# Output of a second feed-forward network with token rows: the hidden tile held, 384 and 192 weight columns moving

## The chip, the cores and the metric

One core of a Trainium2 chip runs the kernel. The metric is the device time of one execution in microseconds, median of several runs. The engines are TensorE (PE, with its weight loads as PEld), VectorE (DVE), ScalarE (ACT), GpSimd (POOL) and SyncE (SP), which issues most DMAs.

## The reference

Eight thousand tokens of 192 channels pass three stages:

```python
# causal mixing, per head: softmax over 7 taps, weighted sum of the last 7 tokens
out = np.einsum('hk,bskhg->bshg', w, x_unf)
# network 1: 192 -> 1536 -> 192
g = x @ w_gate; silu = g / (1 + np.exp(-g)); val = x @ w_val
x = silu * val @ w_out1
# network 2: 192 -> 2048 -> 192
h = x @ w_in
g = np.where(h > 0, h, np.exp(np.minimum(h, 0)) - 1)
out = g @ w_out2          # the stage that the change touches
```

All inputs and outputs are float32: x is (2, 4096, 192), the output (8192, 192).

## The kernel before

The tokens are worked off in 16 chunks of T = 512. Inside the chip everything is channel-major: channels (or hidden units) on the 128 partitions, tokens along the columns. Matmuls use rounded f32 (F32R); to keep f32 accuracy every operand is split into a high part and the rest, a low part, and a product is the sum high x high, low weights x high data and high weights x low data.

A chunk passes two phases. `mix_phase(n)` projects the mixed chunk n into gate and value tiles (12 inner tiles f), and in between runs `down1`, the output of network 1, three tiles behind. `elu_phase(n)` does the same for network 2: 8 iterations j project two of the 16 inner tiles k = 2j, 2j+1, and `down2` follows 4 tiles (LAG2, two iterations) behind; tiles 12 to 15 of a chunk are taken in the first two iterations of the `mix_phase` after the next. So TensorE's program alternates one projection (18 matmuls) with two `down` tiles (20 matmuls). Chunks 2 to 14 are a hardware loop (`Fori`), in which wait values are registers; the others are written out.

All these matmuls use half of the 128 rows of the array, 64 rows deep. They are issued in twos: one on the upper rows (TOP, partitions 0 to 63), one on the lower (LOW), with different weights and different PSUM banks, and the two run side by side.

`down(w, ...)` holds 128 weight columns and moves 512 tokens. Its 192 output channels are a main part of 128 (banks `MAIN_A` from the upper rows, `MAIN_B` from the lower) and a tail of 64. The tail's 64 columns of high weights and 64 of low weights share one 128-column tile `tails`, which gives `TAIL_A` and `TAIL_B`. Per inner tile these are five pairs of matmuls: three with `hid_hi`, two with `hid_lo`:

```python
both(MAIN_A, MAIN_B, main_hi, hi, a, False)
both(MAIN_A, MAIN_B, main_lo, hi, False, False)
both(TAIL_A, TAIL_B, tails, hi, a, False)
pe.wait_ge(lo_sem, lo_count)
both(MAIN_A, MAIN_B, main_hi, lo, False, z)
return both(TAIL_A, TAIL_B, tails, lo, False, z)
```

The hidden tile comes from a chain over the engines: VectorE takes the minimum (L837), ScalarE the exponential (L632), VectorE makes `hidden` (L855), ScalarE its rounded high part `hid_hi` (L647), GpSimd the rest `hid_lo` (L460). `hid_hi` and `hid_lo` are rings of 4 tiles; ScalarE may write one when `down2_done` says that `down2` of four tiles before is through. The banks of the projections are used again after two iterations, when `elu_done` has come.

After the 16th tile the output z of a chunk has to leave its four banks. At f == 1 of the later `mix_phase`, ScalarE copies `TAIL_A` and `MAIN_A` (`copy_z`, L584 and L585), VectorE `TAIL_B` and `MAIN_B` (L759, L760); `down1` of the next chunk waits for the copies. GpSimd adds the halves (`sum_z_tail`, `sum_z_main`, f == 2 and 3), SyncE moves the lower half of the tail to the upper partitions by a DMA (`swap_z`), GpSimd adds that (`fold_z_tail`, f == 6), and VectorE transposes main and tail in blocks of 32 x 32 (`turn_z`, L766 and L769, f == 10 and 11). SyncE then stores six bands of 32 channels (`store_band`, 64 KB each, runs of 128 bytes). SyncE's queue in the loop is `swap_halves(n)`, `load_x(n + 3)`, `cross1(n + 1)`, `swap_z(n - 1)`, `cross2(n)`, `store(n - 1)`, all in order.

The end is written by hand: `last_blocks` orders the last four tiles so that the tails finish first, uses all 128 rows for the main parts of tiles 14 and 15, and folds the tail with one more matmul (`FOLDED`); `finish` on VectorE adds and transposes, and SyncE and ScalarE store three bands each.

## Time and profile before

| what | value |
|---|---|
| time, median of 3 runs | 1212.76 us (1210.73 to 1216.68) |
| profiled execution, its own time | 1211.81 us |
| its span, first to last instruction | 1209.9 us |
| TensorE busy | 1202.1 us, 99% |
| TensorE weight loads busy | 1034.7 us, 86% |
| VectorE / ScalarE / GpSimd busy | 878.5 / 669.6 / 767.1 us |
| granted TensorE clock | 1.0 |

Busy time of an engine is the union of its instructions' records. A matmul's record is longer than its share of the engine, since matmuls overlap: records of 0.39 us follow each other in twos. The timeline merges equal instructions that follow each other; "x6" are six of them, and the start is that of the first. A bracket gives the idle time before a row and what ended it. "PEld" is the weight load that belongs to a matmul; a wait of TensorE sits at the load.

### The profile page before, as it was taken

What the parts mean: (1) busy time and instruction counts of PE and PEld (TensorE: products, weight loads), DVE (VectorE), ACT (ScalarE), POOL (GpSimd) and SP (SyncE); (2) the same over time, 40 slices, a digit from 0 to 9 for tenths busy, and PEclk for the clock granted to TensorE, in tenths of its full rate; (3) what the DMA queues carried; (4) which work ended last, traced back from release to release, by engine and by line L of the source; (5) the groups of instructions that cost most, each with busy time, mean ns of one, the idle gap of its engine ahead of it and who ended that gap; (6) DMA issues with size and microseconds to landing.
All of it is one profiled execution on the core that took longest, in us unless ns stands there. A gap on an engine that the chain in (4) does not pass through costs nothing.

```text
span 1209.9 us, 28143 instructions
## 1 busy us (share of the span) xinstructions
PE 1202.1 (99%) x10274; PEld 1034.7 (86%) x10274; DVE 878.5 (73%) x1180; ACT 669.6 (55%) x1081; POOL 767.1 (63%) x576
## 2 busy tenths in 40 slices
PE   9999999999999999999999999999999999999998
PEld 6999888888888888888888888888888888888886
DVE  7788675886758777686776868768687675886776
ACT  6556555464554645546465554655646555465564
POOL 7787755576655756657665576655656655666565
PEclk9999999999999999999999999999999999999999
DMA  8412011120111202012020120201202011120101
GB/s 180 117 40 45 15 34 33 33 46 22 35 23 33 43 22 41 20 30 43 22 48 22 22 43 22 56 13 22 43 22 56 13 30 35 27 51 21 24 19 31
DMA packets 147343, 45.27 MB, mean 37 GB/s; under 512 B 126512, under 2 KB 136368, under 8 KB 147312
## 3 DMA queue, kind: packets, MB, share of 16 engines
q1 hardware_dynamic: 145200, 44.27, 17.8%
q10 hardware_dynamic: 2112, 0.59, 0.2%
q8 instruction: 20, 0.33, 0.1%
q14 instruction: 11, 0.09, 0.0%
HBM read 16.12 MB, written 6.29 MB: 19 GB/s over the span
## 4 chain that ended last, share of the span: by engine, by line
PE 97%; DVE 1%; POOL 1%; issue 0%; ACT 0%; DVEq 0%; ACTq 0%
PE up L928 54%; PE down L928 42%; POOL hid_lo L460 1%; DVE mixed L898 0%; DVE hidden L855 0%; DVE act L837 0%; POOL up_w_lo L334 0%; ACT L656 0%; POOL y_main L464 0%; POOL halves L464 0%; PE down L1129 0%; DVE mixed L895 0%; DVE taps_head L881 0%; DVE stage L766 0%; DVE stage L781 0%
## 5 line engine op out<-in xcount | busy, mean ns | idle before, releaser
L460 POOL TENSOR_TENSOR hid_lo<-hidden,hid_hi 128x512 fp32r<-128x512 f32 x447 | 608.6, 1374 | 426.9 <-ACT hid_hi L613 255.9
L928 PE MATMUL down<-hid_hi,out_w 64*128 64x512 f32 x2684 | 393.0, 391 | 0.0
L928 PEld LDWEIGHTS down<-hid_hi,out_w 64*128 64x128 f32 x2684 | 270.9, 185 | 43.2 <-issue 0.8
L928 PE MATMUL down<-hid_lo,out_w 64*128 64x512 f32 x1790 | 288.7, 391 | 0.0
L798 DVE TENSOR_TENSOR hidden<-act,up 128x512 f32<-128x512 f32 x191 | 130.5, 683 | 168.3 <-ACT act L596 166.8
L837 DVE TENSOR_SCALAR act<-up 128x512 f32<-128x512 f32 x256 | 164.9, 686 | 105.7 <-PE up L928 105.7
L928 PE MATMUL up<-in_b_hi,up_w_lo 64*128 64x512 f32 x1128 | 231.6, 391 | 0.0
L928 PE MATMUL up<-in_b_lo,up_w_hi 64*128 64x512 f32 x1128 | 231.6, 391 | 0.0
L928 PE MATMUL up<-in_b_hi,up_w_hi 64*128 64x512 f32 x1128 | 231.6, 391 | 0.0
L613 ACT ACTIVATE hid_hi<-hidden 128x512 fp32r<-128x512 f32 x192 | 121.6, 633 | 187.6 <-DVE hidden L798 187.5
L632 ACT ACTIVATE act<-act 128x512 f32<-128x512 f32 x256 | 157.5, 633 | 97.6 <-DVE act L837 96.5
L647 ACT ACTIVATE hid_hi<-hidden 128x512 fp32r<-128x512 f32 x256 | 158.6, 630 | 94.4 <-DVE hidden L855 91.1
L928 PEld LDWEIGHTS down<-hid_lo,out_w 64*128 64x128 f32 x1790 | 181.4, 185 | 28.3
L730 DVE SCALAR_TENSOR_TENSOR mixed<-x_t,taps,mixed 128x512 f32<-128x512 f32 x192 | 205.5, 1109 | 0.0
L596 ACT ACTIVATE act<-up 128x512 f32<-128x512 f32 x191 | 114.3, 599 | 140.0 <-PE up L928 136.5
L855 DVE SCALAR_TENSOR_TENSOR hidden<-act,up 128x512 f32<-128x512 f32 x256 | 168.9, 680 | 29.3 <-POOL hid_lo L460 21.2
L928 PE MATMUL up<-in_a_hi,up_w_hi 64*128 64x512 f32 x786 | 161.6, 392 | 0.2 <-DVE hidden L855 0.2
L928 PE MATMUL up<-in_a_hi,up_w_lo 64*128 64x512 f32 x786 | 161.4, 391 | 0.0
L928 PE MATMUL up<-in_a_lo,up_w_hi 64*128 64x512 f32 x786 | 161.4, 391 | 0.0
L928 PEld LDWEIGHTS up<-in_b_lo,up_w_hi 64*128 64x128 f32 x1128 | 115.2, 185 | 17.8
L928 PEld LDWEIGHTS up<-in_b_hi,up_w_hi 64*128 64x128 f32 x1128 | 115.2, 185 | 17.8
L928 PEld LDWEIGHTS up<-in_b_hi,up_w_lo 64*128 64x128 f32 x1128 | 115.2, 185 | 17.8
(103 smaller groups left out, 810.8 us busy)
## 6 DMA issues: line engine op xcount, KB each, us to landing
x_raw<-x_dram SPq DMA_DIRECT2D x136, 64.0 KB, 2.2
out_dram<-stage SPq DMA_DIRECT2D x93, 64.0 KB, 1.8
in_b_hi<-in_b_hi SPq DMA_DIRECT2D x32, 128.0 KB, 2.3
in_b_lo<-in_b_lo SPq DMA_DIRECT2D x32, 128.0 KB, 2.3
swapped<-halves SPq DMA_DIRECT2D x32, 128.0 KB, 2.3
in_a_hi<-in_a_hi SPq DMA_DIRECT2D x30, 128.0 KB, 2.3
in_a_lo<-in_a_lo SPq DMA_DIRECT2D x30, 128.0 KB, 2.3
stage<-w_out_dram SPq DMA_DIRECT2D x7, 384.0 KB, 3.9
```

The lines of the kernel that those rows point to most:

```text
L460: return pool.tensor_tensor(hid_lo[:, slot, :], hidden[:, s, :], hid_hi[:, slot, :].bitcast(F32), ALU.subtract)
L596: nc.scalar.activation(act[:, f % 2, :], gate_bank(f, n)[:, :], ACT.Silu)\
L613: nc.scalar.activation(hid_hi[:, f % RING, :], hidden[:, f % 2, :], ACT.Copy)\
L632: nc.scalar.activation(act[:, k % 2, :], act[:, k % 2, :], ACT.Exp).then_inc(exp_done, 1)
L647: nc.scalar.activation(hid_hi[:, k % RING, :], hidden[:, k % 2, :], ACT.Copy)\
L730: v.scalar_tensor_tensor(mixed[:, part, :], src, tap, mixed[:, part, :], ALU.mult, ALU.add).then_inc(mix_step, 1)
L798: v.tensor_tensor(hidden[:, f % 2, :], act[:, f % 2, :], val_bank(f, n)[:, :], ALU.mult)\
L837: v.tensor_scalar(act[:, k % 2, :], elu_bank(k)[:, :], 0.0, None, ALU.min)\
L855: v.scalar_tensor_tensor(hidden[:, k % 2, :], act[:, k % 2, :], -1.0, elu_bank(k)[:, :], ALU.add, ALU.max).then_inc(elu_done, 1)
L928: return nc.tensor.matmul(dst, lhsT, rhs, start=start, stop=stop, skip_group_check=True)
```

## The change

Network 2's output is computed the other way round. The hidden tile is held and the weights move: 128 tokens of `hid_hi` or `hid_lo` are the held operand, and the columns that move are 384 (192 high and 192 low weights) for `hid_hi` and 192 (high) for `hid_lo`. The result has tokens as rows. Each of the four banks holds one block of 128 tokens: columns 0 to 191 high weights, columns 192 to 383 low weights times high data.

The upper and the lower rows now add into the same banks, at different times: while the upper rows write block b, the lower write `b_low`. Two inner tiles are taken together, in four turns for the high part and four for the low part. Two turns later rows and banks are exchanged, and TensorE waits on its own semaphore `z_turn` for the end of the matmuls two turns before.

```diff
-            def down2(m, k):
...
-                down(out2_w[:, k, :], k % RING, k == 0, False, lo2_done, N2 * m + k + 1)\
-                    .then_inc(down2_done, 1)
+            def by_tokens(k, data, b, b_low, first=False, last=False):
+
+                w = out2_w[:, k, 0:2 * D] if data is hid_hi else out2_w[:, k, 0:D]
+                cols = slice(0, 2 * D) if data is hid_hi else slice(0, D)
+                start, stop = first and b in (0, 1), last and b in (0, 1)
+                mm(Z[b][:, cols], data[TOP, k % RING, b * P:b * P + P], w[TOP], start, stop)
+                return mm(Z[b_low][:, cols], data[LOW, k % RING, b_low * P:b_low * P + P], w[LOW], start, stop)
+
+            def down2_pair(m, k0):
+                two = (k0, k0 + 1)
+                turns = 4 * (N2 // 2 * m + k0 // 2)
...
+                for turn, (b, b_low) in enumerate(((0, 2), (1, 3), (2, 0), (3, 1))):
+                    if turn >= 2:
+                        pe.wait_ge(z_turn, turns + turn - 1)
+                    for k in two:
+                        pe.wait_ge(hi2_done, N2 * m + k + 1)
+                        end = by_tokens(k, hid_hi, b, b_low, first=k == 0)
+                    if turn < 2:
+                        end.then_inc(z_turn, 1)
+                for turn, (b, b_low) in enumerate(((3, 1), (2, 0), (1, 3), (0, 2))):
+                    if turn >= 2:
+                        pe.wait_ge(z_turn, turns + turn + 1)
+                    for k in two:
+                        pe.wait_ge(lo2_done, N2 * m + k + 1)
+                        end = by_tokens(k, hid_lo, b, b_low, last=k == N2 - 1)
+                    if turn < 2:
+                        end.then_inc(z_turn, 1)
+                end.then_inc(down2_done, 2)
```

`down1` keeps its form; its first tile waits for `result_done` of the last block in place of `z_a` and `z_b`. ScalarE copies the four blocks' low products into `result`, VectorE adds the high ones to them, at the same places where the four copies stood; halves, swap, fold and transposes are gone from GpSimd, SyncE and VectorE. A chunk is stored in one DMA, each row of 768 bytes whole. The low weights of `w_out2` are made in one operation for each piece where there were two.

```diff
+                for b in range(BLOCKS):
+                    nc.scalar.activation(result[:, b, :], Z[b][:, D:2 * D], ACT.Copy).then_inc(z_a, 1)
...
+            def add_z(m):
+                for b in range(BLOCKS):
+                    v.wait_ge(z_a, BLOCKS * m + b + 1)
+                    v.tensor_tensor(result[:, b, :], result[:, b, :], Z[b][:, 0:D], ALU.add)                        .then_inc(result_done, 1)
...
-                for q in range(OUT_BANDS):
-                    store_band(sp, m, q)
+                store_tokens(sp, m)
```

The end: tiles 12 and 13 are a `down2_pair`; tiles 14 and 15 use all 128 rows, one block after the other, and each block is copied, added and stored alone.

```diff
+                down2_pair(CHUNKS - 1, N2 - 4)
+                for b in (0, 1):
+                    for k in two:
+                        whole(b, k, hid_hi)
+                    whole(b, N2 - 2, hid_lo)
+                for b in (0, 1):
+                    whole(b, N2 - 1, hid_lo, True).then_inc(last_z, 1)
+                for b in (2, 3):
+                    for k in two:
+                        whole(b, k, hid_hi)
+                    whole(b, N2 - 2, hid_lo)
+                    whole(b, N2 - 1, hid_lo, True).then_inc(last_z, 1)
```

TensorE's program in the loop, one inner tile of `down2` (down0 to down3 are the banks, the shape is the output's). Before:

```order
L928 MATMUL down0<-hid_hi,out2_w 128x512 [waits hi2_done]
L928 MATMUL down1<-hid_hi,out2_w 128x512
L928 MATMUL down0<-hid_hi,out2_w 128x512
L928 MATMUL down1<-hid_hi,out2_w 128x512
L928 MATMUL down2<-hid_hi,out2_w 128x512
L928 MATMUL down3<-hid_hi,out2_w 128x512
L928 MATMUL down0<-hid_lo,out2_w 128x512 [waits lo2_done]
L928 MATMUL down1<-hid_lo,out2_w 128x512
L928 MATMUL down2<-hid_lo,out2_w 128x512
L928 MATMUL down3<-hid_lo,out2_w 128x512
```

After, from the last high turn into the third low turn of two tiles (L860 is the same helper):

```order
L860 MATMUL down3<-out2_w,hid_hi 128x384 [waits hi2_done]
L860 MATMUL down1<-out2_w,hid_hi 128x384
L860 MATMUL down3<-out2_w,hid_lo 128x192 [waits lo2_done]
L860 MATMUL down1<-out2_w,hid_lo 128x192
L860 MATMUL down3<-out2_w,hid_lo 128x192 [waits lo2_done]
L860 MATMUL down1<-out2_w,hid_lo 128x192
L860 MATMUL down2<-out2_w,hid_lo 128x192 [waits lo2_done]
L860 MATMUL down0<-out2_w,hid_lo 128x192
L860 MATMUL down2<-out2_w,hid_lo 128x192 [waits lo2_done]
L860 MATMUL down0<-out2_w,hid_lo 128x192
L860 MATMUL down1<-out2_w,hid_lo 128x192 [waits lo2_done,z_turn]
L860 MATMUL down3<-out2_w,hid_lo 128x192
```

Where 20 matmuls with four waits stood for two tiles, there are now 32 with 20 waits, four of them on TensorE's own `z_turn`.

VectorE's program in `elu_phase` of the last round (the same pieces stand at f == 1 of every `mix_phase`). Before:

```order
L855 SCALAR_TENSOR_TENSOR hidden<-act,up 128x512 [waits lo2_done,exp_done] x2
L759 COPY stage<-down 128x512 [waits down2_done]
L760 COPY stage<-down 128x512
L837 TENSOR_SCALAR act<-up 128x512 [waits elu_done,h2_ready] x2
L855 SCALAR_TENSOR_TENSOR hidden<-act,up 128x512 [waits lo2_done,exp_done] x2
```

After:

```order
L787 SCALAR_TENSOR_TENSOR hidden<-act,up 128x512 [waits lo2_done,exp_done] x2
L720 TENSOR_TENSOR stage<-stage,down 128x192 [waits z_a] x4
L771 TENSOR_SCALAR act<-up 128x512 [waits elu_done,h2_ready] x2
L787 SCALAR_TENSOR_TENSOR hidden<-act,up 128x512 [waits lo2_done,exp_done] x2
```

Two copies have become four additions, each behind one of ScalarE's copies.

## Rows read from the trace of the kernel before

**Rows 1.** The page, parts 1 and 2: busy shares; busy tenths and granted clock by slice.

```profile
PE 1202.1 (99%) x10274; PEld 1034.7 (86%) x10274; DVE 878.5 (73%) x1180; ACT 669.6 (55%) x1081; POOL 767.1 (63%) x576
...
PEclk9999999999999999999999999999999999999999
```

**Rows 2.** Waits: engine, line <- releaser: us in total, times, longest us.

```profile
DVE hidden L855 <- POOL hid_lo L460: 21.2, 53, 1.3
...
PE up L928 <- DVE hidden L862: 1.3, 1, 1.3
```

**Rows 3.** The chain of waits: shares by line, then its longest pieces (start, us).

```profile
by line: PE up L928 54.3%; PE down L928 42.4%; POOL hid_lo L460 0.6%; issue 0.5%; DVE mixed L898 0.4%; DVE hidden L855 0.2%; DVE act L837 0.2%; POOL up_w_lo L334 0.1%; ACT L656 0.1%; POOL halves L464 0.1%; POOL y_main L464 0.1%; PE down L11
...
1166.15 4.65 PE down L928 x40
```

**Rows 4.** Timeline, last chunk's ELU phase: start, us, engine, line, operation, count.

```profile
1188.05 0.87 PE L928 MATMUL down<-hid_hi,out_w 64*128 64x512 f32 x6
...
1190.38 0.40 PE L928 MATMUL up<-in_b_hi,up_w_hi 64*128 64x512 f32 x2
1190.38 0.20 PEld L928 LDWEIGHTS up<-in_b_hi,up_w_lo 64*128 64x128 f32 x2
...
1194.50 1.24 DVE L855 SCALAR_TENSOR_TENSOR hidden<-act,up 128x512 f32<-128x512 f32 x2
...
1196.89 0.86 PE L928 MATMUL down<-hid_hi,out_w 64*128 64x512 f32 x6
...
1199.20 1.23 ACT L647 ACTIVATE hid_hi<-hidden 128x512 fp32r<-128x512 f32 x2 [0.16 <-DVE hidden L855]
```

**Rows 5.** Timeline, start and last blocks: weight loads (PEld) and the f32 matmuls.

```profile
4.37 0.62 PEld L928 LDWEIGHTS down<-taps_head,head_of 8*128 8x128 f32 x4 [0.48 <-POOL fold L456]
5.09 0.86 PEld L1129 LDWEIGHTS down<-ident,stage 128*128 128x128 f32 x8
...
12.84 0.19 PEld L928 LDWEIGHTS up<-in_a_hi,up_w_hi 64*128 64x128 f32 x2 [0.76 <-issue]
12.95 0.19 PEld L928 LDWEIGHTS up<-in_a_hi,up_w_lo 64*128 64x128 f32 x2
...
7.63 3.67 PE L928 MATMUL down<-hidden,act 128*128 128x512 f32 x8 [1.00 <-ACT act L668]
...
1202.55 0.30 PEld L928 LDWEIGHTS down<-hid_hi,out_w 128*128 128x128 f32 x2 [0.36 <-issue]
```

**Rows 6.** Groups by form: busy us, mean ns; idle before them.

```profile
L928 PE MATMUL down<-hid_hi,out_w 64*128 64x512 f32 x2680 | 391.6, 391 | 0.0
...
L584 ACT ACTIVATE stage<-down 128x512 f32<-128x512 f32 x15 | 9.0, 599 | 6.9 <-PE down L928 6.9
...
L659 ACT ACTIVATE silu_first<-taps_neg 8x1 f32<-8x1 f32 x1 | 0.2, 202 | 0.0
...
L769 DVE STREAM_TRANSPOSE stage<-stage 64x512 f32<-64x512 f32 x15 | 10.5, 697 | 0.0
...
L710 DVE COPY x_t<-halos 128x12 f32 x13 | 2.2, 167 | 0.0
...
L464 POOL TENSOR_TENSOR stage<-stage 128x512 f32<-128x512 f32 x30 | 41.5, 1384 | 0.0
L464 POOL TENSOR_TENSOR stage<-stage 64x512 f32<-64x512 f32 x15 | 25.7, 1713 | 0.0
```

**Rows 7.** Timeline, last blocks: ends of matmuls and adds, and who starts then.

```profile
1203.36 0.69 DVE L778 TENSOR_TENSOR stage<-stage,down 128x512 f32<-128x512 f32 x1 [0.93 <-ACT stage L692]
...
1203.81 0.40 PE L928 MATMUL down<-hid_lo,out_w 128*128 128x512 f32 x1
1204.10 0.30 PEld L928 LDWEIGHTS up<-stage,fold 128*128 128x128 f32 x2 [0.33 <-DVE stage L778]
...
1204.25 0.69 DVE L781 TENSOR_TENSOR stage<-stage,down 128x512 f32<-128x512 f32 x1 [0.21 <-PE down L928]
```

**Rows 8.** Timeline, ScalarE's queue: the last stores.

```profile
1205.72 1.52 ACTq L340 DMA_DIRECT2D out_dram<-stage  x3
```

More of the change, by code:

```diff
@@ L231, in mix_ffn_ffn @@
         last_lo_done = sem("last_lo_done")
+        last_z = sem("last_z")
+        z_turn = sem("z_turn")
         MIX = 2 * TAPS + 2
@@ L335, in make_lo, with store_tokens @@
                 ins.then_inc(piece_lo_dve if who == "dve" else piece_lo_pool, 1)
[L337 to L341 removed]
+        def store_tokens(eng, m, blocks=slice(0, BLOCKS)):
+            eng.dma_start(out_rows[m][:, blocks, :], result[:, blocks, :]).then_inc(stored, 16)
         block = ctx.enter_context(nc.Block())
@@ L420, in _ @@
                 cross1(n + 1)
-                swap_z(n - 1)
                 cross2(n)
@@ L519, in elu_phase @@
                     lo_of(k % 2, k % RING).then_inc(lo2_done, 1)
-                    if k == 3:
-                        sum_z_tail(n - 2) if last else sum_y_tail(n)
-                    if k == 5:
-                        sum_z_main(n - 2) if last else sum_y_main(n)
-                    if k == 9:
-                        fold_z_tail(n - 2) if last else fold_y_tail(n)
+                    if k == 3 and not last:
+                        sum_y_tail(n)
+                    if k == 5 and not last:
+                        sum_y_main(n)
+                    if k == 9 and not last:
+                        fold_y_tail(n)
                     if k % 2:
@@ L800, in mix_phase @@
                     if f == 1 and not (lead and n < 2):
-                        copy_z(n - 2)
-                    if f in (10, 11) and not (lead and n < 2):
-                        turn_z(n - 2, f - 10)
+                        add_z(n - 2)
                     if f == 1 and is_int(n, 0):
@@ L838, in elu_phase @@
                             .then_inc(min_done, 1)
-                    if j in (5, 6) and last:
-                        turn_z(n - 2, j - 5)
                     if j in (5, 6) and is_int(n, CHUNKS - 1):
@@ L857, in elu_phase @@
                     if j == 0:
-                        copy_z(n - 2) if last else copy_y(n)
+                        add_z(n - 2) if last else copy_y(n)
                     extra(j)
@@ new lines, in down2_pair, with whole @@
+                for turn, (b, b_low) in enumerate(((3, 1), (2, 0), (1, 3), (0, 2))):
[7 more added lines that the diff above has]
+                end.then_inc(down2_done, 2)
+            def last_blocks():
+                two = (N2 - 2, N2 - 1)
+                def whole(b, k, data, last=False):
@@ L1009, in tails @@
                     pe.wait_ge(hi2_done, N2 * (CHUNKS - 1) + k + 1)
-                    both(TAIL_A, TAIL_B, w_tails, hi, False, False)
-                    if k == N2 - 1:
+                    if data is hid_lo and k == N2 - 1:
                         pe.wait_ge(last_lo_done, 1)
-                    else:
+                    elif data is hid_lo:
                         pe.wait_ge(lo2_done, N2 * (CHUNKS - 1) + k + 1)
-                    return both(TAIL_A, TAIL_B, w_tails, lo, False, k == N2 - 1)
@@ new lines, in whole @@
+                    cols = slice(0, 2 * D) if data is hid_hi else slice(0, D)
+                    return mm(Z[b][:, cols], data[:, k % RING, b * P:b * P + P], w, False, last)
+                down2_pair(CHUNKS - 1, N2 - 4)
[10 more added lines that the diff above has]
+                    whole(b, N2 - 1, hid_lo, True).then_inc(last_z, 1)
@@ L1101, in elu_phase @@
                     if j == 0 and last:
-                        for k in range(N2 - LAG2, N2):
-                            down2(n - 2, k)
+                        for k in range(N2 - LAG2, N2, 2):
+                            down2_pair(n - 2, k)
                     elif j == 0:
```

154 lines of the change are left out of this document (30 added, 124 removed).

## The prediction

> **What bounds the kernel now.** I read the page's busy shares first [rows 1]: TensorE is busy 1202.1 of 1209.9 us at the full granted clock (1.0, the 2.4 GHz level) and no other engine is above 73%. The waits of TensorE confirm it [rows 2]: its longest wait on another engine is 1.3 us, once. The chain of waits [rows 3] is 54.3% `up` and 42.4% `down` matmuls, and gives the unit of everything below: 40 matmuls of `down` take 4.65 us, so one *step*, an upper-row and a lower-row matmul of 512 columns running side by side, takes 0.2325 us. 512 columns at 2.4 GHz are 0.2133 us, so each step carries 0.019 us beyond its columns. TensorE has no holes, so what is added to its stream between chunk 0 and the end goes to the span one to one; what leaves the other engines gives nothing.
>
> **The change on TensorE.** Per two inner tiles `down2` did 20 matmuls of 512 columns, 10 steps, 10 x 0.2325 = 2.325 us (timeline [rows 4]: 1190.38 - 1188.05 = 2.33 us). There are 16 chunks x 8 = 128 such pairs. Now there are 8 steps of 384 columns and 8 of 192: 4608 columns for 5120, 10% fewer, but 16 steps and 16 weight loads for 10.
>
> *384 columns.* No row has this length. If the 0.019 us belongs to each step, it takes 0.160 + 0.019 = 0.179 us; if the stream as such is slower, 0.2325 x 384/512 = 0.174 us. I take the middle, 0.177: 8 x 0.177 = 1.416 us.
>
> *192 columns.* The columns need 0.080 us, with the 0.019 of a step 0.099. But each step needs its own weight load, and in the timeline the load for a step starts when the step before starts [rows 4]: the loads of the second step and the matmuls of the first are both at 1190.38. It can be no more than one load ahead. A load alone is visible where TensorE had drained [rows 5]: two loads of 187 ns together take 0.30 us, so the second starts 0.11 after the first, and the same at 12.84 and 12.95 for a pair of 64-row loads, which run side by side. In the same rows, eight loads with 128-column transposes take 0.86 us: (0.86 - 0.14)/7 = 0.10; four loads with 7 moving columns (0.62 - 0.19)/3 = 0.14. I take 0.111, the nearest in kind, so the load sets the pace and not the columns: 8 x 0.111 = 0.888 us. Ends: 0.099 and 0.14.
>
> Together 2.304 us for 2.325. **The 10% fewer columns are nearly all lost** to loads that no longer hide and to more steps. The Trainium skill (TensorE: Matmul & The Clock Gate, Back-to-back issue gap) gives columns/2.4 + 2.5 ns for a step, which would make 8 x 0.1625 + 8 x 0.0825 = 1.96 us and save 47 us; at 512 columns it says 0.216 where this trace has 0.2325. The same skill (TensorEngine Tiling (Array Packing), Instruction Overhead) speaks of about 60 cycles for each matmul, against this change: 12 more matmuls per pair would be 0.30 us, 38 us in all; the trace's 0.019 per step does not bear that out.
>
> *The wait on its own matmuls.* In turns 2 and 3 the upper rows write the bank that the lower rows wrote two turns before, so TensorE waits for `z_turn`, set when that turn's last matmul has ended. A 512-column matmul is recorded for 0.391 us [rows 6], 0.213 of it columns, so one of 384 lasts 0.337 and one of 192 0.258. From a matmul's end to the start of VectorE's work on it is 0.04 us (1203.81 + 0.40 to 1204.25), from VectorE's end to the load that waited 0.05 (1203.36 + 0.69 to 1204.10) [rows 7]. I take 0.05. High turns: the load may start at 0.337 + 0.05 = 0.387, the matmul at 0.497; unwaited it would start at 3 x 0.177 = 0.531. Nothing is lost, with 0.034 to spare. Low turns: load at 0.308, matmul at 0.419, unwaited 3 x 0.111 = 0.333: **0.086 us lost**. The wait of turn 3 then finds its turn just ended, so once per pair. Ends: nothing, if the release is quicker than I think, and 0.2, if turn 3 pays too.
>
> *More wait instructions.* 20 waits per pair where there were 4, their values counted in registers inside the loop (13 of the 16 chunks, 104 pairs). In the trace of before such steps hide behind 0.2325 us of columns; behind a 0.111 us load they may not. From nothing to one load, 0.11; I take 0.035.
>
> Sum per pair: 1.416 + 0.888 + 0.086 - 2.325 = +0.065, x 128 = +8.3 us; plus 0.035 x 104 = +3.6 us. **+11.9 us.**
>
> **The other engines, each chunk.** ScalarE copies 4 x 192 columns for 2 x 512: 0.2 fixed (the 8x1 row) plus 0.4 x 192/512 makes 0.35 each, 1.4 us for 1.2 [rows 6]. VectorE adds 4 blocks, about 0.33 each between its 0.17 (12 columns) [rows 6] and 0.69 (512) [rows 7], 1.3 us for two copies and two transposes of some 0.69 each, 2.8. GpSimd loses three sums, 4.5 us [rows 6]. None of it is on the chain. What TensorE waits for is new: `down1` of the next chunk needs `result_done` instead of the two copies. The adds end 0.05 + 1.4 + 0.05 + 0.33 = 1.8 us after the last `down2`; two projections, 18 steps or 4.2 us, lie in between. VectorE stands in this wait some 0.3 us longer than before, with the mixing of the next chunk behind it, and has 1.5 us given back. Cost: nothing. `down2_done` now comes for two tiles at once, and ScalarE's next `hid_hi` waits for it. It started at 1199.20, 2.31 us after that `down2` began [rows 4]; now not before 2.43 - 0.11 + 0.26 + 0.04 = 2.62, so 0.3 us later, and GpSimd's `hid_lo` behind it. TensorE needs these tiles an iteration (19 steps, 4.42 us) later, and a bank that VectorE frees at 1194.50 + 1.24 = 1195.74 is wanted again two iterations after 1190.38, at 1199.2; the 21.2 us in which VectorE waits for GpSimd [rows 2] may grow without reaching TensorE. SyncE loses `swap_z` and 5 of 6 stores per chunk, and rows are written 768 B at a time: it gets less late. The prepared weights lose one small operation for each of four pieces, before TensorE needs them: nothing.
>
> **The end.** TensorE's last part: before, from 1199.21 (1196.89 plus 10 steps, [rows 4]) to 1203.81 + 0.40 = 1204.21 [rows 7]. After: one pair 2.39, the drain on the way to full rows, which the load at 1202.55 shows to exist in both kernels [rows 5], estimated at 0.1, 8 x (0.177 + 0.111) = 2.30; the last matmul starts at 1203.89 and ends at 1204.15, the same. Then copy 0.35, add 0.33 and three hand-overs of 0.05 give the last store at 1204.97. Before, fold, transposes and three stores put the last one at about 1205.72 + 1.52 - 0.5 = 1206.7 (the last third of three in a row, [rows 8]), 3.2 us before the span's end. Gain 1.7 us.
>
> **Sum: +11.9 - 1.7 = +10.2 us.** The profiled execution took 1211.81 us (span 1209.9), 0.95 under the median of 1212.76, so it stands for the median: **1223.0 us**.
>
> **Rivals.** (a) *Waits met for nothing.* If semaphores and registers cost TensorE nothing, the pair is 2.304 us, -0.021 x 128 = -2.7, with the end -4.4: 1208.4; with 0.179 for the long step 1210.4. For it: the release is 0.05 us of guesswork, and the other engines' waits hide well now. Against: 0.333 us is shorter than one matmul's recorded length plus a load.
> (b) *The load does not bind.* If 192 columns go in 0.099 and the waits are free as well, the pair is 1.416 + 0.792 = 2.208, -0.117 x 128 - 1.7 = -16.7: 1196.1. It decides from a pair of 2.29 us down. For it: a long stream may overlap loads better than the drained TensorE of rows 5. Against: a load never starts before the previous step does. The Trainium skill's rule on the gap, above, points the same way.
> (c) *Every turn waits.* If the release takes 0.10 and not 0.05, the two late low turns lose 0.05 more each and the two late high turns 0.016 each: 0.13 x 128 = +17 on top: 1240.
> (d) *Short streams at the plain f32 rate.* Eight f32 records of 512 columns take 3.67 us [rows 5], 0.44 each, two to a product, so 192 columns would take 0.33: 8 x 0.22 x 128 = +225 us, 1448. No row shows a rounded-f32 matmul under 512 columns, so nothing excludes it, and nothing suggests it.
>
> **Chances.** Within 0.5% (6.1 us) is about what a measurement of this kernel can tell from no change. Forecast 0.56, (c) 0.10, (d) 0.03, all slower; (a) 0.17, no change; (b) 0.14, faster. The range is 1205 to 1243 us: it takes in most of the bounds of step and wait costs (a low step of 0.111 + 0.019 = 0.13 us would be 8 x 0.019 x 128 = +19), (a) and (c), and leaves out (b) and (d).
>
> **What would show it.** Right: `down<-out_w,hid_hi` steps 0.175 to 0.18 us apart, `hid_lo` steps 0.11, a TensorE hole of some 0.09 us in the middle of each low half and none in the high half; 2.4 us per pair; last store near 1205 plus the shift. Wrong: low steps at 0.10 or under, no hole (a, b); holes in high turns (c); TensorE waiting for VectorE's adds before `down1`, which I priced at nothing.

## The result and the profile after

The changed kernel takes **1222.3 us** (median of 6 runs, 1220.92 to 1222.49). The kernel before, run beside it, took 1216.68 us (6 runs, 1210.73 to 1217.18). The ratio of after to before is **1.0057, with a 95% interval of 1.0036 to 1.0078**: slower by 0.57%. Each of its runs lies above each of the 31 runs of before in this document (1217.47 us at most). The forecast was 1223.0 us and slower.

One thing has to be known to read this ratio. The kernel before has two levels: four of its six runs lie at 1216.7 to 1217.2 us, two at 1210.7 and 1212.8, and its median falls on either (1212.76 in the first three runs, 1216.68 with six, 1215.79 and 1212.17 beside the experiments). The profiled execution of before, at 1211.81 us, is of the lower level. Profile against profile the change costs 1220.92 - 1211.81 = 9.1 us, where +10.2 was forecast. Runs e3 and b2 below look at the levels, which are no matter of the granted clock (1.0 in both).

The page of after shows TensorE as full as in [rows 1], at the same granted clock in every slice, and the weight loads busier (1079.9 us for 1034.7):

```profile
PE 1213.0 (100%) x11798; PEld 1079.9 (89%) x11798; DVE 787.7 (65%) x1178; ACT 666.9 (55%) x1114; POOL 710.2 (58%) x528
```

The waits of after, TensorE's longest on another engine and ScalarE's for `down2` in the ELU phases (engine, line <- releaser: us in total, times, longest us):

```profile
PE up L860 <- DVE hidden L794: 1.3, 1, 1.3
...
ACT hid_hi L608 <- PE down L860: 20.7, 49, 0.5
```

TensorE waits for no other engine more than once, as in [rows 2]. There is no wait for VectorE's additions (L720): `result_done` comes in time. ScalarE now stands 20.7 us in 49 short waits for `down2_done`, none over 0.5 us. That is the "0.3 us later" of the prediction; 13 more such waits, up to 1.4 us, stand in the mix phases (L574). Nothing of either reaches TensorE.

### One pair of tiles

Timeline of after, last chunk's ELU phase, TensorE's matmuls; it answers to [rows 4]:

```profile
1190.56 1.58 PE L860 MATMUL down<-out_w,hid_hi 64*128 64x384 f32 x16
1191.98 1.12 PE L860 MATMUL down<-out_w,hid_lo 64*128 64x192 f32 x16
1192.93 0.42 PE L860 MATMUL up<-in_b_hi,up_w_hi 64*128 64x512 f32 x2
1193.19 0.39 PE L860 MATMUL up<-in_b_hi,up_w_lo 64*128 64x512 f32 x2
...
1195.05 1.58 PE L860 MATMUL down<-out_w,hid_hi 64*128 64x384 f32 x16
```

And its weight loads at the same place:

```profile
1191.80 1.12 PEld L860 LDWEIGHTS down<-out_w,hid_lo 64*128 64x128 f32 x16
1192.84 0.19 PEld L860 LDWEIGHTS up<-in_b_hi,up_w_hi 64*128 64x128 f32 x2
```

The eight steps of 384 columns take 1191.98 - 1190.56 = 1.42 us, 0.1775 each. The eight of 192 take 1192.93 - 1191.98 = 0.95 us. From the first of their loads to the first load of the projection are 1192.84 - 1191.80 = 1.04 us: eight spacings of 0.111 are 0.89. Of the other 0.15 us some 0.06 belong to the first load, which starts a whole high step (0.176 us) ahead of the second; the rest is one hole. A single low half in the middle of the span shows the hole itself, in two stretches of the weight-load timeline:

```profile
629.89 0.19 PEld L860 LDWEIGHTS down<-out_w,hid_lo 64*128 64x128 f32 x2
...
630.10 0.30 PEld L860 LDWEIGHTS down<-out_w,hid_lo 64*128 64x128 f32 x4
```

The loads of one step start at 629.89, those of the next at 630.10, 0.21 later where 0.11 is the spacing of the others: the wait for `z_turn`, 0.10 us, where the low half goes from its second turn to the third.

A further effect was not in the prediction. Behind the last low step, the first step of the projection takes 1193.19 - 1192.93 = 0.26 us where it takes 0.23 before [rows 4]. The rows of the loads suggest why: at the start of the low half the first load is 0.18 us ahead of its matmul (1191.80 and 1191.98), at its end only 0.09 (1192.84 and 1192.93). The low half uses up this lead, and the projection has to restore it. One iteration, `down2` of a pair and one projection, goes from 4.42 us to 1195.05 - 1190.56 = 4.49.

### The whole span

The chain of before, at four places of the program that both kernels have (start, us, what):

```profile
54.64 6.30 PE up L928 x54
...
206.19 4.18 PE up L928 x36
...
1098.52 4.19 PE up L928 x36
...
1197.06 7.17 PE down L928 x53
```

The chain of after:

```profile
54.34 6.26 PE up L860 x54
...
243.71 4.20 PE up L860 x36
...
1146.08 4.20 PE up L860 x36
...
1208.69 7.27 PE down L860 x80
```

- From the projection at 54 us to the last tiles of the last chunk, before needs 1197.06 - 54.64 = 1142.42 us and after 1208.69 - 54.34 = 1154.35: **+11.9 us**, which is also the forecast for TensorE's stream.
- From there to the end of the span: before 1209.9 - 1197.06 = 12.8, after 1218.9 - 1208.69 = 10.2: **-2.6 us**.
- Ahead of it, 0.3 us less.
- Sum: +9.0 us, the difference of the spans.

The +11.9 holds one wait that only before has: in its first ELU phase TensorE waits once for VectorE (PEld up L928 <- DVE hidden L855, 0.6 us, 118 us into the span), and in after it doesn't.

The loop alone: 12 chunks take 892.33 us before (74.36 each) and 902.37 after (75.20), +0.84 us a chunk. Of this 0.24 us are no part of the change, as run e3 shows. In e3, where the unchanged steps are as quick as in the trace of before, an iteration takes 4.480 us for 4.415 on average, 0.065 more, and eight make 0.52. In each chunk the iteration in which the mix phase begins is 0.08 us longer still (4.57 us in after). Why is open; e1 and e2 don't have it.

The end of after (start, us, engine, line):

```profile
1215.59 0.36 PE L860 MATMUL down<-out_w,hid_lo 128*128 128x192 f32 x2
1215.99 0.33 ACT L654 ACTIVATE stage<-down 128x192 f32<-128x192 f32 x1 [0.24 <-PE down L860]
...
1216.35 0.35 DVE L720 TENSOR_TENSOR stage<-stage,down 128x192 f32<-128x192 f32 x1 [0.22 <-ACT stage L654]
```

ScalarE's copy takes 0.33 us (0.35 forecast) and VectorE's addition 0.35 (0.33). The last matmul ends at 1215.95, the last addition at 1216.70, and the span ends at 1218.9: 2.95 us behind the last matmul, where before took 1209.9 - 1204.21 = 5.7 [rows 7, 8].

### The profile page after: what moved, and what is told of

It is laid out like the page before. It is cut to its first block, busy times and chain, and to the rows that moved or that the text cites. A ratio compares the mean times of both kernels' runs of the same rounds, so it can differ in the third digit from the quotient of the medians.

```text
span 1218.9 us, 31852 instructions
## 1 busy us (share of the span) xinstructions
PE 1213.0 (100%) x11798; PEld 1079.9 (89%) x11798; DVE 787.7 (65%) x1178; ACT 666.9 (55%) x1114; POOL 710.2 (58%) x528
## 4 chain that ended last, share of the span: by engine, by line
PE 99%; DVE 1%; ACT 0%; issue 0%; ACTq 0%; DVEq 0%
PE up L860 55%; PE down L860 44%; DVE mixed L830 0%; ACT L617 0%; PE down L1068 0%; DVE mixed L827 0%; DVE taps_head L813 0%; ACTq L615 0%; DVE stage L720 0%; ACT stage L654 0%; ACT taps_exp L617 0%; DVE taps_inv L812 0%; DVE taps_sum L810 0%; DVE taps_eps L811 0%; DVEq L826 0%
## 5 line engine op out<-in xcount | busy, mean ns | idle before, releaser
L441 POOL TENSOR_TENSOR hid_lo<-hidden,hid_hi 128x512 fp32r<-128x512 f32 x447 | 615.4, 1388 | 495.9 <-ACT hid_hi L574 310.8
L860 PE MATMUL up<-in_b_hi,up_w_hi 64*128 64x512 f32 x1128 | 235.4, 395 | 0.0
L860 PE MATMUL up<-in_b_lo,up_w_hi 64*128 64x512 f32 x1128 | 233.9, 391 | 0.0
L860 PE MATMUL up<-in_b_hi,up_w_lo 64*128 64x512 f32 x1128 | 233.8, 391 | 0.0
L574 ACT ACTIVATE hid_hi<-hidden 128x512 fp32r<-128x512 f32 x192 | 121.6, 633 | 177.4 <-DVE hidden L734 160.2
L860 PE MATMUL down<-out_w,hid_hi 64*128 64x384 f32 x2040 | 204.0, 336 | 0.0
L860 PEld LDWEIGHTS down<-out_w,hid_hi 64*128 64x128 f32 x2040 | 177.8, 184 | 17.5
L860 PE MATMUL down<-hid_hi,out_w 64*128 64x512 f32 x1152 | 172.3, 393 | 0.0
L860 PE MATMUL up<-in_a_hi,up_w_hi 64*128 64x512 f32 x786 | 166.4, 396 | 0.0
L860 PE MATMUL up<-in_a_lo,up_w_hi 64*128 64x512 f32 x786 | 164.7, 391 | 0.0
L860 PE MATMUL up<-in_a_hi,up_w_lo 64*128 64x512 f32 x786 | 164.4, 391 | 0.0
L690 DVE SCALAR_TENSOR_TENSOR mixed<-x_t,taps,mixed 128x512 f32<-128x512 f32 x192 | 146.2, 802 | 0.0
L860 PEld LDWEIGHTS down<-out_w,hid_lo 64*128 64x128 f32 x2040 | 143.2, 186 | 1.5
L860 PE MATMUL down<-out_w,hid_lo 64*128 64x192 f32 x2040 | 144.1, 279 | 0.0
L860 PEld LDWEIGHTS down<-hid_hi,out_w 64*128 64x128 f32 x1152 | 121.8, 184 | 15.8 <-issue 0.4
L860 PEld LDWEIGHTS up<-in_b_lo,up_w_hi 64*128 64x128 f32 x1128 | 116.7, 184 | 17.4
```

Source lines behind the costliest of these rows:

```text
L441: return pool.tensor_tensor(hid_lo[:, slot, :], hidden[:, s, :], hid_hi[:, slot, :].bitcast(F32), ALU.subtract)
L574: nc.scalar.activation(hid_hi[:, f % RING, :], hidden[:, f % 2, :], ACT.Copy)\
L690: v.scalar_tensor_tensor(mixed[:, part, :], src, tap, mixed[:, part, :], ALU.mult, ALU.add).then_inc(mix_step, 1)
L860: return nc.tensor.matmul(dst, lhsT, rhs, start=start, stop=stop, skip_group_check=True)
```

## The experiments

Each kernel is the changed kernel with one edit (b2: the kernel before). The first four ran on one chip, beside 13 runs of before (median 1215.79 us, 1211.43 to 1217.47), the others on a second, beside 11 (1212.17 us, 1210.85 to 1216.85). Because of the two levels of before, medians of the experiments are compared with each other more than with it; where the two came from different chips, the timelines bear the difference out. Spans are compared with care: in all eight profiled executions below the first projection starts at 13.9 to 14.0 us, in those of before and after at 12.84 and 12.65. TensorE's first small matmuls are slower in them. Eight transposes in b2, the kernel before once more:

```profile
5.30 1.97 PE L1129 MATMUL down<-ident,stage 128*128 128x128 f32 x8
```

In before they take 1.10 us, from 5.09. The granted clock is 1.0 in both; what makes the difference stays open.

### e1: no exchange

```diff
-for turn, (b, b_low) in enumerate(((0, 2), (1, 3), (2, 0), (3, 1))):
-    if turn >= 2:
-        pe.wait_ge(z_turn, turns + turn - 1)
+for turn, (b, b_low) in enumerate(((0, 2), (1, 3), (0, 2), (1, 3))):
...
-for turn, (b, b_low) in enumerate(((3, 1), (2, 0), (1, 3), (0, 2))):
-    if turn >= 2:
-        pe.wait_ge(z_turn, turns + turn + 1)
+for turn, (b, b_low) in enumerate(((1, 3), (0, 2), (1, 3), (0, 2))):
```

The upper rows always write banks 0 and 1, the lower rows 2 and 3. Number and length of the matmuls are unchanged, but the products of the exchanged half are left out and others counted twice.

> The changed kernel, but the upper rows always write banks 0 and 1 and the lower rows banks 2 and 3, so no wait on z_turn is needed and none is there. (It sums the wrong blocks: each bank gets only half of the inner channels of its tokens, some twice.) Instructions, columns and weight loads are the same in number. Theory (the wait on TensorE's own matmuls costs 0.09 us once per pair of tiles): the hole in the low half goes, 8 low steps take 0.87 us for 0.95, and the time falls by 128 x 0.09 = 11.5 us to about 1211. Rival 1 (the added wait instructions slow it, not the wait): four of twenty waits go, at most 2 us less. Rival 2 (a low step is dearer by itself): no change, 1222.

Measured: 1208.74 us (1207.91 to 1209.53), ratio to before 0.9945 (0.9925 to 0.9966). That is **13.6 us less than after**, 0.106 for each of the 128 pairs. Its timeline, same place:

```profile
1179.91 1.57 PE L860 MATMUL down<-out_w,hid_hi 64*128 64x384 f32 x16
1181.32 1.03 PE L860 MATMUL down<-out_w,hid_lo 64*128 64x192 f32 x16
1182.19 0.42 PE L860 MATMUL up<-in_b_hi,up_w_hi 64*128 64x512 f32 x2
1182.45 0.39 PE L860 MATMUL up<-in_b_hi,up_w_lo 64*128 64x512 f32 x2
```

The high half takes 1.41 us as in after. The low half takes 0.87 for 0.95: the hole is gone. The late first step of the projection, 0.26, is still there, so it doesn't come from the exchange. The loop says the same without medians: 74.35 us a chunk in e1, 75.20 in after, 0.106 for each pair. The wait on the kernel's own matmuls is the whole reason why the change loses: without it the 16 shorter steps take 2.28 us for the 2.325 of the 10 long ones.

### e2: one exchange for each pair

```diff
-turns = 4 * (N2 // 2 * m + k0 // 2)
+pair = N2 // 2 * m + k0 // 2
...
-for turn, (b, b_low) in enumerate(((0, 2), (1, 3), (2, 0), (3, 1))):
+ways = ((0, 2), (1, 3), (2, 0), (3, 1)) if k0 % 4 == 0 else ((2, 0), (3, 1), (0, 2), (1, 3))
+for turn, (b, b_low) in enumerate(ways):
     if turn >= 2:
-        pe.wait_ge(z_turn, turns + turn - 1)
+        pe.wait_ge(z_turn, 2 * pair + turn - 1)
     for k in two:
+        if turn == 0:
             pe.wait_ge(hi2_done, N2 * m + k + 1)
-        end = by_tokens(k, hid_hi, b, b_low, first=k == 0)
-    if turn < 2:
-        end.then_inc(z_turn, 1)
-for turn, (b, b_low) in enumerate(((3, 1), (2, 0), (1, 3), (0, 2))):
-    if turn >= 2:
-        pe.wait_ge(z_turn, turns + turn + 1)
+        by_tokens(k, hid_hi, b, b_low, first=k == 0)
     for k in two:
+        if turn == 0:
             pe.wait_ge(lo2_done, N2 * m + k + 1)
         end = by_tokens(k, hid_lo, b, b_low, last=k == N2 - 1)
     if turn < 2:
         end.then_inc(z_turn, 1)
```

A block takes its two high and its two low steps in one go, and the next pair begins the other way round. The result is the full product. Between a turn and the one two later there are now two high and two low steps.

> The changed kernel with another order inside a pair of tiles, same result: each block takes its high and its low steps together (high, high, low, low), so rows and banks are exchanged once per pair and not twice, with four steps (0.57 us) between a block's last matmul and the other half's first one into its bank; the next pair starts as this one ended. Each tile's semaphore is waited for once. Theory (exchange too early after short matmuls): the wait finds its matmuls ended, no hole, a pair takes 1.416 + 0.888 = 2.30 us plus 0.02 at the border to the projections, and the time is 1209 to 1211, at or a little under the kernel before. Rival 1 (changing between 384 and 192 columns every two steps costs something): four more such borders per pair, each up to 0.02 us, +10 us, so 1220. Rival 2 (the low parts are wanted earlier now, after two high steps, and GpSimd is late): waits of TensorE for GpSimd appear, over 1222.

Measured: 1206.95 us (1205.67 to 1207.05), ratio to before **0.9931 (0.9913 to 0.9949)**, 15.4 us less than after. Timeline of e2, the last block of a pair and the border to the projection:

```profile
1174.73 0.53 PE L860 MATMUL down<-out_w,hid_hi 64*128 64x384 f32 x4
1175.10 0.36 PE L860 MATMUL down<-out_w,hid_lo 64*128 64x192 f32 x4
1175.30 0.42 PE L860 MATMUL up<-in_b_hi,up_w_hi 64*128 64x512 f32 x2
1175.55 0.39 PE L860 MATMUL up<-in_b_hi,up_w_lo 64*128 64x512 f32 x2
```

The block takes 1175.30 - 1174.73 = 0.57 us, 0.37 for its high and 0.20 for its low steps. The other three blocks take the same, with no hole at the exchange, and four make the 2.28 us of e1. The exchange of banks costs nothing where one turn is 0.57 us long, more than a matmul's record and a release. That it is 1.8 us below e1 is taken up with e3. Rival 2 shows in the first ELU phase alone, where GpSimd still prepares weights: one wait of TensorE for `hid_lo`, 0.3 us at 122 us, behind one of 0.4 for VectorE. With these waits that phase is 1.3 us longer than the later ones.

### e3: the waits once

```diff
                     for k in two:
-                        pe.wait_ge(hi2_done, N2 * m + k + 1)
+                        if turn == 0:
+                            pe.wait_ge(hi2_done, N2 * m + k + 1)
```

The same for `lo2_done`: 8 waits per pair for 20. The matmuls and `z_turn` stay.

> The changed kernel, but hi2_done and lo2_done are waited for once per tile and not in every turn: 8 waits per pair for 20, z_turn stays. Theory (the sequencer's extra instructions cost almost nothing; in the trace low steps with a register operation between them are 0.108 to 0.114 us apart, as those without): 0 to 1 us less than 1222. Rival (they cost the 0.035 us per pair that the prediction put on them): 3.6 us less, 1218.5.

Measured: 1222.33 us (1218.5 to 1222.53), ratio to before 1.0058 (1.0039 to 1.0078); after had 1222.3. By the medians the 12 waits cost nothing. The profiled execution is the lowest of e3's runs, 1218.5 us, which happens to be the rival's number, and its chunk is 74.95 us (899.44/12) for 75.20. But the difference lies where nothing was changed. Five iterations of projection and `down1`, a stretch that the kernels have in common, in the chain of e3:

```profile
288.15 2.09 PE up L860 x18
...
304.42 1.62 PE up L860 x13
```

and in after:

```profile
287.20 2.10 PE up L860 x18
...
303.54 0.47 PE up L860 x4
```

They last 16.27 us in e3 and 16.34 in after, 0.001 us for each of their 5 x 14 steps. A chunk has 240 such steps outside `down2` (20 projections of 9, 12 tiles of `down1` of 5), which makes 0.24 of the 0.25 us. What is left to the wait and register instructions is 0.01 us a chunk, where 0.28 was forecast: nothing that can be seen. e1 and e2 say the same. e1 has the slower steps (16.33 us for these five iterations) and e2 the quicker (16.27), which is 0.20 of the 0.21 us between their chunks, although e2 has 10 waits fewer in each pair (6 for 16). So the two levels are in the changed kernels as well; after's profiled execution has the slower steps, and that of before has the quicker.

### e4: low steps of 96 columns

```diff
-                cols = slice(0, 2 * D) if data is hid_hi else slice(0, D)
+                cols = slice(0, 2 * D) if data is hid_hi else slice(0, D // 2)
```

This is e1 with half of the low product's columns left out; the number of steps and loads is the same.

> As e1_no_exchange, but the low steps move 96 columns and not 192 (the other half of the low product is left out). Theory (the weight load sets the pace of a low step, 0.111 us, whatever moves): time as e1_no_exchange within 1.5 us. Rival (columns plus a fixed 0.019 to 0.03 us set the pace): 0.04 us less per low step, 8 x 0.04 x 128 = 41 us less than e1_no_exchange, about 1170.

Measured: 1206.63 us (1205.48 to 1206.79), **2.1 us less than e1**, a little outside the 1.5 us expected, where half of the low columns at the speed of the high ones would have been over 40. Its timeline:

```profile
1181.40 1.63 PE L860 MATMUL down<-out_w,hid_hi 64*128 64x384 f32 x16
1182.81 1.05 PE L860 MATMUL down<-out_w,hid_lo 64*128 64x96 f32 x16
1183.63 0.53 PE L860 MATMUL up<-in_b_hi,up_w_hi 64*128 64x512 f32 x2
```

Eight steps of 96 columns take 0.82 us, eight of 192 took 0.87. But the projection behind them is longer by as much, and a whole iteration takes 4.39 us in both kernels. Nor are the 2.1 us won by the columns: e4 has the quicker steps (its five unchanged iterations take 16.27 us, those of e1 16.33, see e3), which makes 0.2 us a chunk and some 3 us in all. So half of the columns gives back nothing. The weight load sets the pace of a low step, as the prediction had it. Only the first low step of a half, whose load has a high step to hide behind, goes at the pace of its columns: 0.087 us on average over e1's low halves, where 192 x 0.459 ns are 0.088.

The Trainium skill (TensorE: Matmul & The Clock Gate, Back-to-back issue gap) gives columns/2.4 + 2.5 ns for a matmul by itself, and says that at small widths this leaves out the weight load. Taken for these steps it would have made e4 8 x 0.04 x 128 = 41 us quicker than e1. This trace agrees with that caveat: with a load for each matmul a low step takes 0.11 us and not 0.0825.

### e6: high steps of 256 columns

```diff
-                w = out2_w[:, k, 0:2 * D] if data is hid_hi else out2_w[:, k, 0:D]
-                cols = slice(0, 2 * D) if data is hid_hi else slice(0, D)
+                w = out2_w[:, k, 0:2 * P] if data is hid_hi else out2_w[:, k, 0:D]
+                cols = slice(0, 2 * P) if data is hid_hi else slice(0, D)
```

On e1 again; a third of the high product is left out. It measures how a long step depends on its columns.

> As e1_no_exchange, but the high steps move 256 columns and not 384 (a third of the high product is left out). It prices a step's length: 512 columns take 0.2324 us, 384 take 0.1765. If what is beyond the columns belongs to the step (0.017 to 0.019), 256 columns take 0.124 and the time is 8 x 0.0525 x 128 = 54 us under e1_no_exchange, 1155. If it is in proportion to the columns, 0.118 and 60 us less, 1149. A line through the two known lengths gives 0.1206 and 57 us less, 1151.5. If the load of 0.11 us binds here already, the high steps stay over 0.126 and it is 1157 or more.

Measured: 1149.0 us (2 runs, 1148.45 and 1149.55), ratio to before 0.9464 (0.9433 to 0.9495), 59.7 us less than e1. Its timeline:

```profile
1122.24 1.11 PE L860 MATMUL down<-out_w,hid_hi 64*128 64x256 f32 x16
1123.18 1.03 PE L860 MATMUL down<-out_w,hid_lo 64*128 64x192 f32 x16
1124.05 0.42 PE L860 MATMUL up<-in_b_hi,up_w_hi 64*128 64x512 f32 x2
```

A step of 256 columns takes (1123.18 - 1122.24)/8 = 0.1175 us, one of 384 columns 0.176 (e1), one of 512 columns 0.2325 [rows 3]. These are 0.459, 0.459 and 0.454 ns a column. So nearly all of the 0.019 us "beyond its columns" grows with the columns: what is left as a fixed part is 2 x 0.1175 - 0.2325 = 0.0025 us. The time alone doesn't decide it. e6 has the quicker steps and e1 the slower (16.27 and 16.33 us for five unchanged iterations), some 3 us of the 59.7, and 57 us less was the forecast of the line through the two known lengths, not of the proportion; the steps of the timeline decide.

### e8: low steps first

```diff
     for k in two:
         if turn == 0:
+            pe.wait_ge(lo2_done, N2 * m + k + 1)
+        by_tokens(k, hid_lo, b, b_low, first=k == 0)
+    for k in two:
+        if turn == 0:
             pe.wait_ge(hi2_done, N2 * m + k + 1)
-        by_tokens(k, hid_hi, b, b_low, first=k == 0)
-    for k in two:
-        if turn == 0:
-            pe.wait_ge(lo2_done, N2 * m + k + 1)
-        end = by_tokens(k, hid_lo, b, b_low, last=k == N2 - 1)
+        end = by_tokens(k, hid_hi, b, b_low, last=k == N2 - 1)
```

On e2. A pair now ends on a high step, so that the load of the projection's first step has 0.177 us to hide behind, not 0.111. The result is the full product.

> As e2_one_exchange, but in each block the two low steps come before the two high ones, so a pair of tiles ends with a step of 384 columns and not with one of 192. Theory (the step after a low one waits for its weight load: behind a pair the first projection step is 0.02 us late, eight times a chunk): the border cost goes, projections take 0.2324 us a step again, 128 x 0.02 = 2.6 us less than e2_one_exchange, about 1204.4. Rival 1 (the border costs nothing, the longer projections have another cause): as e2_one_exchange, 1207. Rival 2 (the low parts are now the first thing wanted, GpSimd makes them last): TensorE waits for GpSimd, 1209 and more.

Measured: 1205.19 us (1202.93 to 1205.88), ratio to before **0.9924 (0.9903 to 0.9945)**, the fastest kernel with the full product. Against e2 it is 1.8 us less in the median (on another chip) and 2.5 us in the spans of the profiled executions (1202.6 for 1205.1); 1.3 us of the 2.5 are the waits of e2 in its first ELU phase, which e8 doesn't have. Timeline of e8, a projection's first steps, and the first of the next projection:

```profile
1181.48 0.39 PE L860 MATMUL up<-in_b_hi,up_w_hi 64*128 64x512 f32 x1
...
1181.65 0.39 PE L860 MATMUL up<-in_b_hi,up_w_hi 64*128 64x512 f32 x1
1181.71 0.57 PE L860 MATMUL up<-in_b_hi,up_w_lo 64*128 64x512 f32 x2
...
1185.85 0.39 PE L860 MATMUL up<-in_b_hi,up_w_hi 64*128 64x512 f32 x1
```

The next step of the first half of the rows follows 1181.71 - 1181.48 = 0.23 us behind, not 0.26, and the iteration is 1185.85 - 1181.48 = 4.37 us for 4.39 in e2. The two halves of the rows no longer start together but 0.17 us apart (1181.48 and 1181.65), which wasn't expected. So the late first step is gone. What comes back in all is less than its 0.02 to 0.03 us: a chunk of the loop takes 74.03 us for the 74.13 of e2, 0.013 us for each pair, 1.7 us over 128. e8 shows that this much can be had back; that it is the hiding of the load alone, and not the new distance between the halves as well, is argued and not shown.

### e5: all 128 rows

```diff
+for data, made in ((hid_hi, hi2_done), (hid_lo, lo2_done)):
+    w = 2 * D if data is hid_hi else D
+    for b in range(BLOCKS):
+        for k in two:
...
+            end = mm(Z[b][:, 0:w], data[:, k % RING, b * P:b * P + P], out2_w[:, k, 0:w], ...)
```

Each step is one matmul over all rows: 16 for a pair instead of 32, no exchange and no wait for one. The result is the full product.

> The changed kernel, same result, but every matmul of a pair of tiles uses all 128 rows: 16 matmuls of the same lengths for 32, no exchange of banks, no z_turn. Theory (a change between 64 and 128 rows drains TensorE and leaves a load uncovered; in the last blocks of the kernel before it took 0.32 us for a 0.23 us step, and the first load 0.11 more): two such changes per pair, about 0.4 us for both, so 128 x 0.4 = 51 us over e2_one_exchange, 1240 to 1260. Rival (the drain hides behind other work and only the row halves' wait mattered): 1207, as e2_one_exchange.

Measured: 1252.71 us (1251.5 to 1253.15), ratio to before 1.0316 (1.0289 to 1.0344). Its timeline around a pair:

```profile
1226.15 0.40 PE L860 MATMUL up<-in_b_lo,up_w_hi 64*128 64x512 f32 x2
1226.47 1.68 PE L860 MATMUL down<-out_w,hid_hi 128*128 128x384 f32 x8
1227.99 1.03 PE L860 MATMUL down<-out_w,hid_lo 128*128 128x192 f32 x8
1228.95 0.50 PE L860 MATMUL up<-in_b_hi,up_w_hi 64*128 64x512 f32 x2
1229.29 0.39 PE L860 MATMUL up<-in_b_hi,up_w_lo 64*128 64x512 f32 x2
```

The last step of the projection lasts 0.32 us, 0.09 more than its 0.2325. The high half takes 1.52 us for 1.41, the low half 0.96 for 0.87, and the first step of the next projection 0.34, 0.08 more than in e1. Together 0.37 us a pair, 47 us over 128 pairs: the 44.0 us between e5 and e1. Inside the pair the steps keep their pace (0.175 us for the high ones, 0.11 for the low ones, in the trace's single starts); what is added stands at the borders. The whole-row form has no hazard of its own, but pays for going from 64 rows to 128 and back. The Trainium skill (TensorEngine Tiling (Array Packing)) says under its key properties that a change of mode drains TensorE; this trace agrees, with about 0.19 us for each change. The two row halves with their exchange are the cheaper form.

### b2: before once more

> The kernel before, unchanged, for a second trace. Its times spread from 1210.7 to 1217.5 us while each other kernel stays within 2 us. If this execution is near 1217, its trace shows where the 5 us are: in every step of 512 columns (0.2335 us and not 0.2324), or in single waits. If it is near 1211, nothing follows.

Measured: 1216.76 us, span 1214.9, the upper level. Its chain of waits, 12 chunks:

```profile
244.19 3.50 PE up L928 x30
...
1140.19 3.50 PE up L928 x30
```

A chunk is 896.00/12 = 74.67 us for 74.36, and a step takes 0.2333 us (3.50/15) for 0.2325. The timeline shows what else is different:

```profile
351.11 0.39 PE L928 MATMUL up<-in_b_hi,up_w_hi 64*128 64x512 f32 x1
351.14 0.39 PE L928 MATMUL down<-hid_hi,out_w 64*128 64x512 f32 x1
...
351.37 0.40 PE L928 MATMUL down<-hid_lo,out_w 64*128 64x512 f32 x1
...
351.60 0.39 PE L928 MATMUL down<-hid_lo,out_w 64*128 64x512 f32 x1
351.81 0.42 PE L928 MATMUL up<-in_b_hi,up_w_hi 64*128 64x512 f32 x2
```

At the lower level the two matmuls of a step start together ("x2" in one row, [rows 4]). Here one half of the rows starts its projection at 351.11, when the other still has three matmuls of `down` to do (351.14, 351.37, 351.60); it begins its own projection as the second matmul of the last row. It is 0.72 us behind, three steps and 0.02 us. This lag grows through the trace, from 0.03 us at 28 us over 0.18 at 95 to 0.72 at 228 us, and stays there. While it grows the first half needs 3.2535 us for an iteration of 14 steps and the second 3.2665, 0.2324 and 0.2333 us a step; from 228 us on both need the longer one. So the two levels are two paces, each half of the rows has its own, and once the lag is three steps the slower half sets the pace of both.

The lag goes with the levels in this trace but doesn't make them. e1 has the slower pace with its halves 0.003 us apart, e4 and e8 have the quicker one with theirs 0.07 and 0.17 us apart. And in half of the mix phases of after one half has the quicker pace and the other the slower. Two rows of after, early and late in one such phase:

```profile
287.04 0.40 PE L860 MATMUL up<-in_b_hi,up_w_hi 64*128 64x512 f32 x2
...
307.25 0.49 PE L860 MATMUL up<-in_b_hi,up_w_hi 64*128 64x512 f32 x2
```

Both rows are two matmuls of one step. In the later one they start 0.09 us apart, and the next exchange of `down2` brings the halves together again.

Of the 5.0 us between b2 and before, 1.1 stand ahead of the first projection (13.92 for 12.84 us); the rest are the steps, 0.31 us in each of 13 chunks. What gives a half of the rows the slower pace in one execution and not in the next stays open.

## Why the prediction was right

The verdict was right, by the mechanism forecast, and the time as well: 1222.3 for 1223.0 us. In the trace TensorE's stream grows by +11.9 us, as forecast, with -2.6 at the end and -0.3 at the start for -1.7. But this closeness is in part luck: a term of +3.6 us was wrong, and 3 us that are not the change's own stand in its place. Level against level the change costs 1222.3 - 1216.7 = 5.6 us (the two medians, both at the upper level) or 1218.5 - 1211.8 = 6.7 (profiled executions of e3 and before, 1.1 of it for the later first projection of e3), not 10.2.

- **The 384-column step, 0.177 us: right** (0.1775; 0.176 in e1). The value lay between two models. e6 decides for the second in the main, a stream that is slower as such: 0.459 x 384 = 0.176.
- **The 192-column step bound by its load, 0.111 us: right.** Loads follow each other by 0.11, and e4 shows that halving the columns gives back nothing: its 2.1 us are less than what its quicker steps make elsewhere. Rival (b), that the load does not bind, falls with this; the Trainium skill's rule that it leaned on is one for a matmul without a load (e4). The two rows that were nearest in kind, two loads of a drained TensorE 0.11 us apart [rows 5], were the right ones.
- **The wait on its own matmuls, 0.086 us once in each low half, none in the high half: right.** The hole is 0.10 us, once, and e1 removes 13.6 us where 0.086 x 128 = 11.0 and the `z_turn` instructions stood. Rivals (a), waits met for nothing, and (c), every turn waits, fall. The hole of 0.10 makes the release 0.064 us where the guess was 0.05.
- **Wait and register instructions, 0.035 x 104 = +3.6 us: wrong.** e3 leaves nothing of them, and e1 against e2 neither. Without this term the forecast would have been +6.6 us, near what level against level gives. The step that failed was to take a price from the middle between nothing and a load where no row showed one.
- **The border to the projection: missing.** The prediction priced the pair and let the next projection begin with a full 0.2325 us step. It takes 0.26: 0.025 x 128 = +3.2 us. For it the low half came out 0.024 us shorter than forecast, 0.95 for 0.888 + 0.086 = 0.974, since it lives on the lead of its loads. The two cancel: at like pace an iteration costs 0.065 us more (e3 against before), which is the pair's sum. One iteration in each chunk costs 0.08 us on top, about 1 us in all, and was not foreseen. Of the late first step, e8 shows that 0.013 us a pair can be had back.
- **The level of the steps: missing.** 0.24 us a chunk on 240 unchanged steps, +3.1 us over the 13 chunks of the loop. The three first times of before, 1210.73 to 1216.68, spoke of it, and the prediction took the profiled execution for the median without asking what lay between. Against it stands the one wait of 0.6 us that only before has.
- **The end, -1.7 us: too small**, -2.6. The last matmul and the copy and addition behind it came as forecast (0.33 and 0.35 us). The store wasn't: the span ends 2.2 us behind the last addition (1218.9 - 1216.70), where "3.2 us before the span's end" was taken from before for the last of three queued stores. ScalarE's stores land 1.7 us after their issue in after (96 KB, rows of 768 bytes) and 2.6 in before (64 KB, runs of 128 bytes, three in a row). Whether it is the queue or the longer rows that makes the last one quicker, no run separates.
- **The other engines: right.** None of their terms shows in TensorE's waits.
- **Rival (d)**, the plain f32 rate for short streams, falls by a wide margin: 0.11 us for the 0.33.

What made the change a loss is one term, +0.10 us a pair by a wait that the order of the turns makes necessary. e2 and e8 keep all the rest of the change, move the exchange to where it finds its banks free, and are faster than both kernels, by 1.4% than after (1205.19/1222.3) and by 0.76% than before; the slowest run of e8, 1205.88 us, lies below the quickest of before, 1210.73, so that the levels of before don't matter here.

## What to carry to other kernels

Before moving the narrow operand instead of the wide one, compare the columns of the new step with the time between two weight loads (0.11 us here, an estimate of 240 columns at 0.459 ns): below it, fewer columns gain nothing, and each step also leaves the next, longer one without cover. Where two streams take turns at the same accumulator, count the time between writer and next writer in steps and let long and short steps alternate (2 high + 2 low = 0.57 us), so that a matmul's full recorded length plus its release, 0.06 us here, fits into every turn and not only into the mean. End a stretch of short steps on a long one.

## What was not expected of the hardware

- A step's cost is nearly in proportion to its columns: 0.459 ns a column at 256 and 384, 0.454 at 512, against 0.417 at 2.4 GHz. A fixed part that fewer steps could save is no more than some 0.003 us by these three lengths.
- Each half of the rows has a pace of its own, 0.2324 or 0.2333 us for a step of 512 columns at the same granted clock. The slower one makes the upper level of the kernel before (b2), and the changed kernels have both paces as well (e3).
- The halves need not run together: in b2 one lags 0.72 us, three steps, behind the other. In e8 they run 0.17 us apart at no loss.
- Going from half of the rows to all of them and back costs 0.37 us a pair of changes (e5).
